# Eleven ring slots, quartered w_in and w_out loads, and new engine orders for the first token group

## The reference

```python
# attention: q, k, v (4, 8, 576, 64), window of 128, slope per head
scores = where(mask, q @ k.T / 8 - slope * rel, -1e9);  x = softmax(scores) @ v   # -> (2304, 512)
# mixture of 8 experts with 4 slots each
logits = x @ phi                                   # (2304, 32)
slot_input = softmax(logits, axis=0).T @ x         # (32, 512)
slot_out[e] = relu(slot_input[e] @ w1[e]) @ w2[e]  # w1 (8, 512, 1024), w2 (8, 1024, 512)
y = softmax(logits, axis=1) @ slot_out             # (2304, 512)
# feed-forward: w_in (512, 2048), w_out (2048, 512)
h = relu(y @ w_in);  out = (h * h) @ w_out
```

## Time and profile before

| | us |
|---|---|
| median of 3 runs | 444.12 |
| lowest and highest | 441.32, 444.37 |
| the profiled execution, own time | 441.98 |
| its span | 440.1 |
| TensorE busy in the span | 407.3 (93%) |
| VectorE, ScalarE, GpSimd busy | 239.9, 218.4, 71.6 |
| DMA | 61.35 MB, mean 139 GB/s |

### The profile page before, as it was taken

One profiled execution on the slowest core, in us unless ns is written; L12 is line 12 of the kernel. 1 busy time (PEld: TensorE's weight loads), 2 busy tenths in 40 slices (PEclk: granted clock), 3 DMA queues, 4 the chain that ended last, 5 costly groups with the idle time before them and its releaser, 6 DMA issues.

```text
span 440.1 us, 7853 instructions
## 1 busy us (share of the span) xinstructions
PE 407.3 (93%) x2851; PEld 309.3 (70%) x2851; DVE 239.9 (55%) x678; ACT 218.4 (50%) x557; POOL 71.6 (16%) x61
## 2 busy tenths in 40 slices
PE   4799999898988988955999999999999999999996
PEld 3578787777767553311378888888888888888884
DVE  3888888787844443100499645455445545455520
ACT  2889898888853310000595434434444434444420
POOL 2374756464630010000000000000000000000000
PEclk9999999999999999987799999999999999999999
DMA  8799989999347969999300101010010101010101
GB/s 163 190 248 243 269 214 278 242 276 230 76 124 255 419 212 392 406 386 387 125 1 2 48 1 48 1 48 0 1 49 1 48 0 48 0 48 0 49 0 48
DMA packets 73410, 61.35 MB, mean 139 GB/s; under 512 B 58784, under 2 KB 58784, under 8 KB 71328
## 3 DMA queue, kind: packets, MB, share of 16 engines
q1 hardware_dynamic: 71264, 60.37, 45.0%
q10 hardware_dynamic: 2112, 0.52, 0.7%
HBM read 56.16 MB, written 4.72 MB: 138 GB/s over the span
## 4 chain that ended last, share of the span: by engine, by line
PE 76%; DMA 10%; DVE 4%; SPq 4%; ACT 4%; issue 1%; DVEq 0%
PE psum L1192 15%; PE psum L1190 15%; PE psum L1191 15%; DMA q_in<-in_q 6%; PE psum L934 4%; PE psum L1174 4%; DMA ring_late<-in_moe_w 4%; PE psum L976 3%; PE psum L958 3%; ACT probs L752 3%; PE psum L1099 3%; PE psum L1120 2%; PE psum L1028 2%; PE psum L904 2%; PE psum L1070 1%; PE psum L1160 1%
## 5 line engine op out<-in xcount | busy, mean ns | idle before, releaser
L1190 PE MATMUL psum<-wout_hi,act_hi 128*128 128x512 f32 x288 | 112.8, 392 | 0.0
L1192 PE MATMUL psum<-wout_hi,act_lo 128*128 128x512 f32 x288 | 112.8, 392 | 0.0
L1191 PE MATMUL psum<-wout_lo,act_hi 128*128 128x512 f32 x288 | 112.4, 390 | 0.0
L708 DVE TENSOR_TENSOR sq_h<-relu_h 128x512 f32<-128x512 f32 x72 | 49.8, 692 | 80.8 <-ACT relu_h L859 80.6
L859 ACT ACTIVATE relu_h<-psum 128x512 f32<-128x512 f32 x72 | 43.0, 598 | 91.2 <-PE psum L1174 87.3
L462 POOL TENSOR_TENSOR probs<-probs,row_inv 128x1024 f32<-128x1024 f32 x31 | 59.2, 1928 | 55.9 <-DVE row_inv L553 55.9
L752 ACT ACTIVATE probs<-probs,row_min 128x256 f32<-128x256 f32 (+1 forms) x128 | 60.0, 470 | 13.9 <-DVE row_min L503 13.9
L1192 PEld LDWEIGHTS psum<-wout_hi,act_lo 128*128 128x128 f32 x288 | 54.1, 188 | 11.7
L1191 PEld LDWEIGHTS psum<-wout_lo,act_hi 128*128 128x128 f32 x288 | 54.4, 189 | 8.9
L1190 PEld LDWEIGHTS psum<-wout_hi,act_hi 128*128 128x128 f32 x288 | 54.0, 188 | 9.0
L712 DVE TENSOR_TENSOR act_lo<-sq_h,act_hi 128x512 fp32r<-128x512 f32 x72 | 49.9, 693 | 5.4 <-ACT act_hi L862 0.6
(11 more groups left out here) (128 smaller groups left out, 411.6 us busy)
## 6 DMA issues: line engine op xcount, KB each, us to landing
ring<-in_moe_w SPq DMA_DIRECT2D x13, 1024.0 KB, 6.2
ring<-in_moe_w SPq DMA_DIRECT2D x5, 2048.0 KB, 15.9
ring_late<-in_moe_w SPq DMA_DIRECT2D x3, 2048.0 KB, 14.4
out_x<-out_sb SPq DMA_DIRECT2D x9, 512.0 KB, 2.8
q_in<-in_q SPq DMA_DIRECT2D x32, 128.0 KB, 5.7
v_in<-in_v SPq DMA_DIRECT2D x32, 128.0 KB, 4.2
win_sb<-in_moe_w_in SPq DMA_DIRECT2D x4, 1024.0 KB, 10.6
wout_raw<-in_moe_w_out SPq DMA_DIRECT2D x4, 1024.0 KB, 15.5
```

The lines of the kernel that those rows point to most:

```text
L708: nc.vector.tensor_tensor(sq_h[:, u % 2, :], relu_h[:, u % 2, :], relu_h[:, u % 2, :], ALU.mult).then_inc(sq_done, 1)
L1190: mm(to, hi, wout_hi[:, c, :], start=first_of, stop=False)
L1191: mm(to, hi, wout_lo[:, c, :], start=False, stop=False)
L1192: last = mm(to, lo, wout_hi[:, c, :], start=False, stop=last_of)
```

## The change

- The ring gets eleven slots: seven in `ring` (loaded in halves beside pairs 1 to 14), two in `ring_late` (slots 7 and 8), two in `ring_x` (slots 9 and 10), which lies where `xT` was. `spare` is gone. Item 7 is loaded after the last pair, items 9 and 10 as token rows are turned (`xt_done` 8 and 16), item 8 when all tokens are used, items 11 to 15 each when item i-11 has been used.
- w_in is loaded after the last item, in quarters of columns with rows of 2 KB instead of row groups; w_out comes in quarters between them. `win_sb` now lies where items 9 and 10 were, `wout_raw` where items 7 and 8 were, `combT` and `mix` at the end of `ring`.
- The combine transposes start at expert step 4 instead of 2.
- The slot outputs are read contiguously for `soT` (w_in's rows are grouped accordingly).
- All four quarters of `mix` use banks 6 and 7, and the orders of `first` and of the first step are rewritten on TensorE, ScalarE and VectorE.

```diff
--- before.py
+++ after.py
@@ -28,11 +28,11 @@
 BIG = 3.0e38
 EPS = 1e-9
 KC1 = F1 // P
-RING, RW = 8, 4096
-EARLY = 6
+COMB_FROM = 4
+RING, RW = 11, 4096
+EARLY = 7
+LATE, IN_X = (7, 8), (9, 10)
 ITEMS = 2 * E
-LATE_ITEMS = (8, 10, 12, 9, 14, 11, 13, 15)
-SPLIT_ITEM = 8
 FT = 256
 NFT = NTOK // FT
 FC = F2 // P
@@ -68,7 +68,7 @@
     phi_v = phi.rearrange("(c p) s -> p c s", p=P)
     w1_v = w1.rearrange("e (p c) f -> e p (c f)", c=DC)
     w2_v = w2.rearrange("e (a n) d -> e n a d", n=P)
-    win_v = w_in.rearrange("(p c) f -> c p f", c=DC)
+    win_v = w_in.rearrange("(c p) f -> p c f", c=DC)
     wout_v = w_out.rearrange("(a n) d -> n a d", n=P)
     out_v = out.rearrange("(n t p) d -> n p t d", t=2, p=P)
 
@@ -109,20 +109,19 @@
         ring = sb("ring", [P, EARLY, RW])
         ring_end = place["at"]
         place["at"] = ring_at
-        wout_raw = sb("wout_raw", [P, FC, DM])
-        place["at"] = ring_at
         wout_lo = sb("wout_lo", [P, FC, DM], F32R)
         wout_hi = sb("wout_hi", [P, FC, DM], F32R)
         act_hi = sb("act_hi", [P, FC, FT], F32R)
         act_lo = sb("act_lo", [P, FC, FT], F32R)
-        assert place["at"] == ring_end
-
-        spare = sb("spare", [P, RW // 2])
-
+        mix = sb("mix", [P, F2], F32R)
+        combT = sb("combT", [P, NTOK], F32R)
+        assert place["at"] >= ring_end
 
         xT_at = place["at"]
         xT = sb("xT", [P, DC * NTOK])
         xT_end = place["at"]
+        place["at"] = xT_at
+        ring_x = sb("ring_x", [P, len(IN_X), RW])
         place["at"] = xT_at
         win_sb = sb("win_sb", [P, DC, F2])
         hid = sb("hid", [P, 2, 2 * P])
@@ -328,7 +324,11 @@
             return first + 16 * (i // RING)
 
         def ring_slot(slot):
-            return ring[:, slot, :] if slot < EARLY else ring_late[:, slot - EARLY, :]
+            if slot < EARLY:
+                return ring[:, slot, :]
+            if slot in LATE:
+                return ring_late[:, LATE[1] - slot, :]
+            return ring_x[:, slot - IN_X[0], :]
 
         def load_item(eng, i):
             e, slot = i // 2, i % RING
@@ -337,8 +337,7 @@
                 eng.wait_ge(e2_done if was % 2 else e1_done, was // 2 + 1)
             to = ring_slot(slot)
             if i % 2 == 0:
-                cols = slice(RW // 2 if i == SPLIT_ITEM else 0, RW)
-                eng.dma_start(to[:, cols], w1_v[e][:, cols]).then_inc(ring_loaded[slot], 16)
+                eng.dma_start(to, w1_v[e]).then_inc(ring_loaded[slot], 16)
             else:
 
                 halves = ((0, KC1, ring_loaded[slot]),) if i < ITEMS - 1 else (
@@ -398,23 +397,38 @@
                     load_v(n)
                 if n + 3 < NP:
                     load_k(n + 3)
-                if n < 2 * EARLY:
-                    load_half(n // 2, n % 2)
+                if 1 <= n <= 2 * EARLY:
+                    load_half((n - 1) // 2, (n - 1) % 2)
                 if n + 4 < NP:
                     load_q(n + 4)
-            sp.dma_start(spare[:, :], w1_v[SPLIT_ITEM // 2][:, 0:RW // 2]).then_inc(spare_loaded, 16)
             sp.wait_ge(pv_done, NP)
-            for i in range(EARLY, RING):
+            load_item(sp, LATE[0])
+            for x, slot in enumerate(IN_X):
+                sp.wait_ge(xt_done, 2 * B * (x + 1))
+                load_item(sp, slot)
+            sp.wait_ge(x_used, QT)
+            load_item(sp, LATE[1])
+            for i in range(RING, ITEMS):
                 load_item(sp, i)
-            for c in range(DC):
-                sp.wait_ge(xt_done, B * (c + 1))
-                sp.dma_start(win_sb[:, c, :], win_v[c]).then_inc(win_loaded[c], 16)
-            for i in LATE_ITEMS:
-                load_item(sp, i)
-            sp.wait_ge(e2_done, 5)
-            for i in range(4):
+
+            def load_win(n):
+                cols = slice(512 * n, 512 * n + 512)
+                sp.dma_start(win_sb[:, :, cols], win_v[:, :, cols]).then_inc(win_loaded[n], 16)
+
+            def load_wout(i):
                 sp.dma_start(wout_raw[:, 4 * i:4 * i + 4, :], wout_v[:, 4 * i:4 * i + 4, :]
                              ).then_inc(wout_loaded[i], 16)
+
+            sp.wait_ge(e1_done, IN_X[1] // 2 + 1)
+            sp.wait_ge(e2_done, IN_X[0] // 2 + 1)
+            load_win(0)
+            load_win(1)
+            load_wout(0)
+            load_win(2)
+            load_wout(1)
+            load_win(3)
+            load_wout(2)
+            load_wout(3)
 
             def store(n, par):
                 sp.wait_ge(outA_ready, n + 1)
@@ -666,10 +680,11 @@
                     psum[:, (2, 7)[t % 2], :].rearrange("p (j x) -> p j x", x=P)[:, :, 0:rows]
                     ).then_inc(combT_ready, 1)
 
-            for e in range(2, E):
-                take_hidT(e)
-                if e - 2 < QT:
-                    take_combT(e - 2)
+            for e in range(2, E + 2):
+                if e < E:
+                    take_hidT(e)
+                if 0 <= e - COMB_FROM < QT:
+                    take_combT(e - COMB_FROM)
 
             def split_low(u):
 
@@ -695,12 +710,6 @@
                 dst = mix[2 * NS:P, 512 * n:512 * n + 512]
                 nc.vector.tensor_tensor(dst, psum[2 * NS:P, MIX_BANKS[n][1], :], dst.bitcast(F32), ALU.subtract
                                         ).then_inc(mix_ready, 1)
-
-            take_part(1)
-            split_low(0)
-            take_mix(0)
-            take_mix(1)
-
 
             def low_part(m, u):
 
@@ -715,22 +724,34 @@
                                         ).then_inc(lo_done, 1)
 
             def first():
+                take_mix(0)
+                take_part(1)
                 low_part(0, 0)
-                take_part(3)
-                take_mix(2)
+                split_low(0)
+                take_mix(1)
                 low_part(1, 1)
                 split_low(1)
-                low_part(2, 2)
-                take_mix(3)
-                split_low(2)
-                low_part(3, 3)
-                split_low(3)
 
             def step(n, par):
-                for u in range(AHEAD, FU):
-                    if isinstance(n, int) and n == 0:
-                        split_low(u)
-                    low_part(FU * n + u, u)
+                if isinstance(n, int) and n == 0:
+                    low_part(2, 2)
+                    low_part(3, 3)
+                    take_mix(2)
+                    split_low(2)
+                    split_low(3)
+                    low_part(4, 4)
+                    low_part(5, 5)
+                    take_part(3)
+                    take_mix(3)
+                    split_low(4)
+                    low_part(6, 6)
+                    split_low(5)
+                    low_part(7, 7)
+                    split_low(6)
+                    split_low(7)
+                else:
+                    for u in range(AHEAD, FU):
+                        low_part(FU * n + u, u)
                 if not isinstance(n, int) or n < NFT - 1:
                     for u in range(AHEAD):
                         low_part(FU * (n + 1) + u, u)
@@ -846,13 +867,6 @@
                 act.wait_ge(mix_done, n + 1)
                 nc.scalar.copy(mix[:, 512 * n:512 * n + 512], psum[:, MIX_BANKS[n][1], :]).then_inc(mixhi_ready, 1)
 
-            take_part(0)
-            split_high(0)
-            take_mix(0)
-            split_high(1)
-            take_part(2)
-            take_mix(1)
-
             def high_part(m, u):
                 act.wait_ge(l1_done, m + 1)
                 since(act, sq_done, m - 1)
@@ -864,21 +878,34 @@
                                      ).then_inc(hi_done, 1)
 
             def first():
+                take_part(0)
+                take_mix(0)
                 high_part(0, 0)
+                split_high(0)
+                take_mix(1)
                 high_part(1, 1)
-                take_mix(2)
-                split_high(2)
-                high_part(2, 2)
-                take_mix(3)
-                high_part(3, 3)
-                split_high(3)
-                split_high(4)
+                split_high(1)
 
             def step(n, par):
-                for u in range(AHEAD, FU):
-                    if isinstance(n, int) and n == 0 and u + 1 < FU:
-                        split_high(u + 1)
-                    high_part(FU * n + u, u)
+                if isinstance(n, int) and n == 0:
+                    high_part(2, 2)
+                    high_part(3, 3)
+                    take_part(2)
+                    take_mix(2)
+                    split_high(2)
+                    split_high(3)
+                    high_part(4, 4)
+                    high_part(5, 5)
+                    take_mix(3)
+                    split_high(4)
+                    high_part(6, 6)
+                    split_high(5)
+                    high_part(7, 7)
+                    split_high(6)
+                    split_high(7)
+                else:
+                    for u in range(AHEAD, FU):
```

(68 more changed lines are left out.)

9 lines of the change are left out of this document (3 added, 6 removed).

## The result

The changed kernel takes 447.28 us (median of 10 runs, 443.43 to 451.51) against 443.74 (10 runs, 441.32 to 444.91): a ratio of 1.0079, with a 95% interval of 1.0048 to 1.0110. Part of the 7.5 us between the two spans is therefore chance, and the mean granted clock says where: over the ten executions of the changed kernel it runs from 0.967 to 0.984, and the profiled one has the lowest value, 0.967. (Two of the ten lie more than 1.5% above the fastest; without them the median is 446.86 us, 0.7% above the kernel before.)

What follows compares the result with a forecast made beforehand. DMA was taken to bound the experts, TensorE the dense stretch from 221.7 us. Terms -1.9 - 12.6 - 0.95 + 11.2 + 5.0 gave +0.8 us, 442.8 on the profiled run; stated 443.5, range 438.3 to 449.

Steps and rivals of the forecast that it cites:

- The four waits: First token group: projections 0, 2, 4 and 5 wait 2.4, 3.1, 3.1 and 3.6 us for VectorE's split low.
- the 240 to 250 us: End of the first token group; ending before 240 or after 250 us would show the forecast wrong.
- Attention, -1.9: Attention: half items from pair 1 leave 1 MB less ahead of each q load; 1.9 us saved, bounds 0 and 2.7.
- Experts, -12.6: Expert stage: waits for weights and comb rows go, except 0.5 us charged for item 14; 12.6 us saved.
- fold, -0.95: Slots to soT: contiguous instead of strided weight reads in the fold products; 0.95 us saved, bounds 0 and 0.95.
- Loads for mixing, no wait: First token group: every w_in and w_out piece lands before its first use, w_out 0 by 2 us.
- First group, +11.2 at the full clock: First token group: the new orders cost 11.2 us at the full clock, some 10 of it in four waits.
- The clock, +5.0: First token group: half clock behind TensorE's waits costs 5.0 us, bounds 0 and 9.6.
- the light start: Start of the first token group with its 2.4 us wait: 0.8 us charged for the lower clock.
- The three waits that I priced at 1.4 each: Before projections 2, 4 and 5: waits of 3.1 to 3.6 us, each costing 1.4 us more through the lower clock.
- Rival C: First token group: clock stays half long after waits at projections 2, 4 and 5; +7.3 us, 449.3 in all; chance 0.20.
- the forecast 0.50: Whole kernel: the terms hold as summed, within 3 us of no change, 440.5 to 446 us; chance 0.50.

Runs made afterwards that it cites:

- e1: The changed kernel with the engine orders and mixing banks of the kernel before in the first token group; 431.59 us, ratio 0.9763.
- e9: e6 with extra matmuls, read by nobody, ahead of projections 0, 2, 4 and 5; 438.24 us, ratio 0.9874 to the kernel before.
- e6: The changed kernel with item 14 issued ahead of item 13, nothing else; 444.26 us, ratio 0.9992 to the kernel before.
- e3: The kernel before with only the new orders and mixing banks of the first token group; 460.74 us, ratio 1.039.
- e8: The kernel before with the combine transposes at expert steps 4 to 8 instead of 2 to 6; 445.39 us, ratio 1.0025.

## Why the prediction was wrong

The stated time was 443.5 us, the same as before, with +0.8 us as the sum; measured is +3.5. The four waits and what releases them came as forecast. What was off is the size of several terms, above all the price of the lower clock at the start of the group. The group ended at 253.7, outside the 240 to 250 us that I had named as the sign of being wrong. By the steps of the sum:

- **Attention, -1.9.** The two profiles at hand give -1.7, and the means of four and seven profiles -3.2. Undersized by the means: in the four profiles with halves from pair 0 TensorE's waits for q are 2.7, 7.1, 5.2 and 3.6 us, and the one I had was the shortest.
- **Experts, -12.6, and fold, -0.95.** From siT to soT the two profiles differ by 11.9 instead of 13.55, and over all profiles the kernels with the old loads need 50.3 to 52.0, those with the new ones (item 14 in its old place) 40.1 to 43.3: about 9.4. I charged item 14 with 0.5 us; it was 1.4 to 3.2 late. In the changed kernel's profile it landed as forecast (184.9, seen 185.0), but siT came 1.7 us earlier than in that working, and I let the loads have this head start too. They did not have it: item 12 went out at 165.85, forecast 166.3. A fall of the clock among the fold products, which made the first two in products 1.3 us longer (4.93 against 3.66), is the likely reason; no run separates it. The fold term itself was right, 1.0.
- **Loads for mixing, no wait.** They were later than forecast: e1's quarters 2 and 3 of w_in released TensorE at 203.4 and 208.8, forecast 201 and 206.6. It cost the changed kernel nothing, since its order asks for them only at 212.1 and 224.9.
- **First group, +11.2 at the full clock.** Right to within a microsecond: e9 shows 47.5 us for the forecast 46.6, with the waits at the four places named.
- **The clock, +5.0.** This is the term that failed, in the part for the light start. Three profiles have the new orders without added products, and e9 has the same stretches at the full clock. Starts of the rows shown, subtracted (us):

| | e9 | changed | e6 | e3 |
|---|---|---|---|---|
| first mix part to projection 0 | 8.45 | 10.80 | 10.30 | 10.26 |
| to projection 2 | 11.23 | 12.60 | 12.84 | 11.26 |
| to projection 4 | 11.68 | 13.28 | 13.12 | 13.29 |
| to projection 5 | 6.84 | 8.45 | 6.87 | 6.88 |
| to the dense stretch | 9.26 | 12.08 | 11.75 | 10.86 |
| lost to the clock | | 9.75 | 7.42 | 5.09 |

  The three waits that I priced at 1.4 each, 4.2 together, cost 6.0, 4.0 and 3.2 (rows three to five): right on the average, some of them followed by no fall at all, and the last by up to 2.8. For the start of the group with its wait before projection 0 I had put 0.8, and it cost 3.7, 3.5 and 1.8 (rows one and two). The clock was half for about 6.9 us there in the changed kernel (0.57 in the window of eight), and fell again behind the wait of 2.28, which I had given no fall of its own. That is 1.0 to 2.9 us too little, against the 2.7 that the sum was off. On top of it the profiled execution had a fall at every place. The longest is the one before projection 5, with the half clock for all twelve products, which start every 0.43 us instead of 0.23:

```profile
242.22 0.63 PE L1211 MATMUL psum<-wout_lo,act_hi 128*128 128x512 f32 x1
242.65 0.63 PE L1212 MATMUL psum<-wout_hi,act_lo 128*128 128x512 f32 x1
...
248.00 0.40 PE L1211 MATMUL psum<-wout_lo,act_hi 128*128 128x512 f32 x1
```

  The Trainium skill ("TensorE: Matmul & The Clock Gate", "Why this matters for your kernels") warns of idle gaps between bursts. The trace agrees in part: the falls behind the waits of about 3 us are such. But the waits of 2.97 us before projection 4 in e6 and e3 cost 0.03 and 0.04, and in the changed kernel the clock fell at about 196.6 us with no gap over 0.81 us since 192, while in e9 the same start kept the full clock. Why it falls there in one execution and not in another stays open.

Rival C had the nearest number, +7.3: too high for the median and right for the profiled execution (+7.5). That agreement is partly luck. It took no attention gain, where there was 1.7, and put the loss behind projections 2, 4 and 5, each a whole projection long, with 1.5 for the start; that happened behind projection 5 alone (2.8 and 2.5 us in two of three profiles), and the rest lay at the start of the group. I gave it 0.20, and the forecast 0.50.

The loads of the changed kernel ran at 387 GB/s in the window from 196 to 204 us. The figure of 358 GB/s that I took from the Trainium skill ("DMA: Bandwidth & Descriptors", "Bandwidth") is, by the same section, a core's share when both cores of a pair stream; for one core alone it gives up to 425. This kernel runs on one core, and its 387 agrees with the second.

## What to carry to other kernels

An order written to follow late loads must still put each engine's possible work first: laid out by hand, a first group's four waits came out to 0.2 us before any run. A wait of about 3 us on TensorE can cost more than itself: here 0 to 1.6 us more, and up to 2.8 behind the longest. Price a start of small pieces and short waits in the same way; it was the part I left almost free. And one profile is one draw: the same orders lost 5.1, 7.4 and 9.8 us to the clock in three profiles, so where a stretch waits on DMA or may lose the clock, compare it over all profiles of kernels that share it.

## What the runs showed of the hardware

- The granted clock fell not only in idle stretches: in the changed kernel it was 1.00 from 151 to 155 us, fell in the course of eight fold products of 32 columns that kept TensorE busy for 2.08 us, with 0.87 us idle ahead of them, and was 0.50 at 156.4. In the kernel before, the same products (2.05 us, 0.88 idle ahead) left it at 1.00. With other products in the waits it stayed at 1.00 (e9, 196 to 252 us).
- Reading 128x128 f32 weights at every fourth element cost 2.05 us for eight products (kernel before, 155.70 us), contiguously 1.08 (e9, 193.88 us), both at the full clock.
- The same load list ended attention anywhere within 4 us: in the profiles of the kernel before, e3 and e8 siT was copied at 157.8, 160.8 and 161.8 us, with waits for q of 2.7, 5.2 and 7.1 us in all.
